# Attention and FFN on one core: batch one in a new order, its last 64 keys by two pairs, its sums in a scores bank

## The reference

```python
# q, k, v: (4, 12, 448, 64); x: (1792, 768); w_in: (768, 2048); w_out: (2048, 768); all float32
scores = cap * tanh(q @ k.T / sqrt(64) / cap)
attn = exp(scores - max(scores)); attn = attn / (sum(attn) + 1e-9)
x = (attn @ v), heads side by side            # 1792 tokens x 768
h = relu(x @ w_in); g = s * h * h + b
y = g @ w_out
```

## Time and profile before

| | |
|---|---|
| median of 3 runs | 629.79 us (629.72 to 630.93) |
| the profiled execution | 629.54 us, of which the span is 627.8 |
| busy: PE, DVE, ACT, POOL | 619.4 (99%), 332.0, 258.2, 53.9 us |
| PE in the span's 40 slices, tenths | 8 8 9 9 ... 9 8 |
| chain that ended last, by engine | PE 93%, DVE 3%, ACT 2%, issue 2% |
| KB of one load: lead (in two), q_k, v (with v_tail), w_in | 292 + 160, 448, 192 + 64, 256 |

### The profile page before, as it was taken

How to read it: one execution, slowest core, us unless ns; L and a number is a source line. 1 busy time by engine, 2 the same in 40 slices (tenths; PEclk the granted TensorE clock), 3 DMA queues, 4 the chain that set the end, 5 groups by cost and what they waited for, 6 DMA issues and landing times.

```text
span 627.8 us, 8231 instructions
## 1 busy us (share of the span) xinstructions
PE 619.4 (99%) x3230; PEld 482.7 (77%) x3230; DVE 332.0 (53%) x559; ACT 258.2 (41%) x272; POOL 53.9 (9%) x52
## 2 busy tenths in 40 slices
PE   8899999999999999999999999999999999999998
PEld 5234766667777777777779999999988888888997
DVE  2898899998677767677673233322411122111221
ACT  6885555666464646464513232222411121111220
POOL 4702624500000000000000000000000000000000
PEclk9999999999999999999999999999999999999999
DMA  8522344333322222231014211123432224111501
GB/s 264 155 89 76 109 154 149 100 97 108 105 78 100 75 87 89 73 90 58 29 45 145 75 51 51 55 69 104 152 88 67 68 94 141 48 34 33 172 2 64
DMA packets 31863, 57.17 MB, mean 91 GB/s; under 512 B 3536, under 2 KB 18000, under 8 KB 31824
## 3 DMA queue, kind: packets, MB, share of 16 engines
q1 hardware_dynamic: 31824, 56.64, 28.5%
HBM read 40.11 MB, written 16.52 MB: 90 GB/s over the span
## 4 chain that ended last, share of the span: by engine, by line
PE 93%; DVE 3%; ACT 2%; issue 2%; ACTq 0%; DVEq 0%
PE banks L465 13%; PE banks L467 13%; PE banks L466 13%; PE banks L482 12%; PE banks L483 12%; PE banks L481 12%; PE banks L423 7%; PE banks L378 5%; PE banks L337 2%; PE banks L435 1%; PE banks L403 1%; ACT e L610 1%; DVE e_sum L698 1%; PE banks L491 1%; DVE e_sum L691 1%
## 5 line engine op out<-in xcount | busy, mean ns | idle before, releaser
L465 PE MATMUL banks<-x_hi,w_hi 128*128 128x448 f32 x384 | 142.8, 372 | 0.0
L467 PE MATMUL banks<-x_hi,w_lo 128*128 128x448 f32 x384 | 140.7, 367 | 0.0
L466 PE MATMUL banks<-x_lo,w_hi 128*128 128x448 f32 x384 | 140.6, 366 | 0.0
L482 PE MATMUL banks<-x_lo,w_hi 128*128 128x512 f32 (+2 forms) x384 | 139.4, 363 | 0.0
L483 PE MATMUL banks<-x_hi,w_lo 128*128 128x512 f32 (+2 forms) x384 | 139.4, 363 | 0.0
L481 PE MATMUL banks<-x_hi,w_hi 128*128 128x512 f32 (+2 forms) x384 | 139.4, 363 | 0.0
L774 DVE SCALAR_TENSOR_TENSOR x_lo<-e,beside,x_hi 128x512 fp32r<-128x512 f32 (+1 forms) x48 | 32.5, 684 | 115.4 <-ACT x_hi L624 115.4
L465 PEld LDWEIGHTS banks<-x_hi,w_hi 128*128 128x128 f32 x384 | 72.1, 188 | 14.3 <-issue 8.3
L624 ACT ACTIVATE x_hi<-e,beside 128x512 fp32r<-128x512 f32 (+1 forms) x48 | 31.7, 669 | 116.7 <-PE banks L483 116.7
L482 PEld LDWEIGHTS banks<-x_lo,w_hi 128*128 128x128 f32 x384 | 72.1, 188 | 9.0
L481 PEld LDWEIGHTS banks<-x_hi,w_hi 128*128 128x128 f32 x384 | 72.1, 188 | 9.0
(11 more groups left out here) (62 smaller groups left out, 545.1 us busy)
## 6 DMA issues: line engine op xcount, KB each, us to landing
hidden_scratch<-hidden_sb SPq DMA_DIRECT2D x48, 224.0 KB, 1.9
beside<-q_k SPq DMA_DIRECT2D x23, 448.0 KB, 4.0
e<-hidden_scratch SPq DMA_DIRECT2D x32, 256.0 KB, 2.7
work<-w_in SPq DMA_DIRECT2D x24, 256.0 KB, 4.5
e<-w_out SPq DMA_DIRECT2D x16, 384.0 KB, 3.0
v_sb<-v SPq DMA_DIRECT2D x24, 192.0 KB, 2.5
y_t<-beside SPq DMA_DIRECT2D x10, 256.0 KB, 2.2
e<-hidden_scratch SPq DMA_DIRECT2D x16, 160.0 KB, 2.2
```

Source lines behind the costliest of these rows:

```text
L465: nc.tensor.matmul(out, w_hi[:, j, w], x_hi[:, batch % 2, c, :], start=c == 0, stop=False)
L466: nc.tensor.matmul(out, w_hi[:, j, w], x_lo[:, batch % 2, c, :], start=False, stop=False)
L467: last = nc.tensor.matmul(out, w_lo[:, j, w], x_hi[:, batch % 2, c, :], start=False, stop=c == CT - 1)
L482: nc.tensor.matmul(out, w_hi[:, j, w], ring(x_lo, n), start=False, stop=False)
```

## The change

The order of batch one changes; the later batches compute as before.

- `tail_values` takes a quad (two pairs) and runs only for odd p; `pv_done` counts quads. Even pairs are scaled one iteration later.
- `sums` writes bank 0 of the scores. It waits for `first_tanh(p + 1)` (bank 0 is read) and not for `x_done`; `values` waits for no sums. In exchange tile 0 of the scores of pair p + 2 waits for the sums to be read (`sums_read`); for even pairs tile 1 is made ahead of it.
- The first two hidden chunks of batch one go ahead of the sums of pair 5.
- DVE splits weight pieces 0 to 5, which now have six places (two in `hidden_sb`); POOL makes `x_hi` of batch one and begins with pieces 6 to 9 after it. In DVE's list `x_lo` stands apart from the scaling and mostly behind the transpose; the inversion stands behind the next pair's first add.
- SP's list has pieces 0 and 1 ahead of v, pieces 2 to 5 ahead of q and k of pair 2.
- `WARM_UP` goes from 25 to 13.

```diff
-WARM_UP = 25
+WARM_UP = 13
-        def sums_out(p):
-            return pv[:, (p + 1) % 2, 0:S]
+        def sums_out():
+            return scores[:, 0, 0:S]
         def products(p):
-            return p + 1 if p < PAIRS else PAIRS + (p - PAIRS) // 2 + 1
+            return p // 2 + 1
...
             def load_w_in(piece):
-                reach(sp, w_in_lo, piece - 3)
+                if piece >= CT:
+                    sp.wait_ge(w_in_lo, piece - CT + 1 if piece < CT + 4 else piece - 3)
...
             load_qk(1)
-            load_v(0)
             load_w_in(0)
             load_w_in(1)
+            load_v(0)
+            for piece in range(2, CT):
+                load_w_in(piece)
             load_qk(2)
-            load_w_in(2)
-            load_w_in(3)
             load_v(1)
             load_v(2)
-            load_w_in(4)
             load_qk(3)
-            load_w_in(5)
-            load_w_in(6)
+            for piece in range(CT, CT + 4):
+                load_w_in(piece)
             load_v(3)
...
-                if p <= PAIRS:
-                    for head in range(2 if p else 0):
+                if p <= PAIRS and p % 2 == 0:
+                    for head in range(2):
+                        last = row_scores(p, head, 1, 2 + head)
+                    if p > 0:
+                        pe.wait_ge(sums_read, p - 1)
+                        for head in range(2):
+                            last = row_scores(p, head, 0, head)
+                elif p <= PAIRS:
+                    reach(pe, sums_read, p - 1)
+                    for head in range(2):
                         row_scores(p, head, 0, head)
-                    if p % 2 and p > 1:
+                    if p > 1:
                         pe.wait_ge(last_read, last_group(p - 1))
...
             def values(p):
-                reach(pe, sums_read, min(p, PAIRS))
...
             def sums(p):
-                reach(pe, x_done, p)
+                pe.wait_ge(first_read, first_group(p + 1))
...
                 values(p)
-                tail_values(p, 1)
+                if p % 2:
+                    tail_values(p // 2)
                 if p % 2 and p + 1 < PAIRS:
                     pe.wait_ge(first_read, first_group(p + 1))
                     tail_scores((p + 1) // 2, 2)
+                if p + 1 == PAIRS:
+                    for c in range(2):
+                        hidden_chunk(0, c)
                 sums(p)
-            for c in range(CT - 1):
+            for c in range(2, CT - 1):
                 hidden_chunk(0, c)
             pe.wait_ge(first_read, first_group(PAIRS))
+            pe.wait_ge(sums_read, PAIRS)
...
-            add_first_e(0)
+            for piece in range(4):
+                if piece == 2:
+                    add_first_e(0)
+                w_in_high(piece)
+                w_in_low(piece)
             for p in range(PAIRS):
                 add_last_e(p)
                 if p == 0:
+                    w_in_high(4)
+                    w_in_low(4)
                     dve.wait_ge(guard_done, 2)
-                else:
-                    scale_pair(p - 1)
+                if p % 2:
+                    scale(p - 1)
+                elif p > 0:
+                    x_low(p - 1)
+                turn_first(p)
+                if p % 2:
+                    x_low(p - 1)
                 add_first_e(p + 1)
-                invert_first(p)
-            scale_pair(PAIRS - 1)
+                invert_rest(p)
+                if p == 0:
+                    w_in_high(5)
+                    w_in_low(5)
+                if p % 2:
+                    scale(p)
+            x_low(PAIRS - 1)
...
             def low(piece):
-                pool.wait_ge(w_in_hi, piece + 1)
+                pool.wait_ge(w_in_hi, max(piece + 1, CT + 4))
...
-            for piece in range(CT):
-                high(piece)
-                low(piece)
-            for piece in range(CT, CT + 4):
-                high(piece)
-
-            pool.wait_ge(x_done, PAIRS)
+            for p in range(PAIRS):
+                pool.wait_ge(x_done, p + 1)
+                nc.gpsimd.tensor_copy(x_hi[:, 0, p, :], xt[:]).then_inc(x_hi_done, 1)
+
+            pool.wait_ge(w_in_lo, CT)
+            pool.wait_ge(x_hi_done, PAIRS)
+            for piece in range(CT, CT + 4):
+                high(piece)
             for piece in range(CT, CT + 4):
                 low(piece)
```

More of the change, by code:

```diff
@@ L124, in attention_ffn @@
         v_tail_in = [sem(f"v_tail_in{i}") for i in range(2)]
-        w_in_in = [sem(f"w_in_in{i}") for i in range(4)]
+        w_in_in = [sem(f"w_in_in{i}") for i in range(CT)]
         w_out_in = [sem(f"w_out_in{i}") for i in range(W_RAW)]
@@ L209, in hidden_tile, with w_in_place, w_in_loads, w_in_raw @@
             return hidden_sb[:, n % 3, :] if n < (B - 1) * JT else work[:, n % 4, 0:S]
+        def w_in_place(piece):
+            return piece if piece < CT else (piece - CT) % 4
+        def w_in_loads(piece):
+            return 16 * (1 if piece < CT else 2 + (piece - CT) // 4)
+        def w_in_raw(piece):
+            place = w_in_place(piece)
+            raw = work[:, place, :] if place < 4 else first_raw[:, place - 4, :]
+            return raw
+        def w_in_of(tensor, piece):
+            f, c = divmod(piece, CT)
+            return tensor[:, f * JPP:(f + 1) * JPP, c * P:(c + 1) * P]
         def y_acc(c):
@@ L425, in values, with tail_values @@
                 last.then_inc(main_done, 1)
[L427 to L432, removed]
+            def tail_values(quad):
+                i = quad % 2
+                pe.wait_ge(v_tail_in[i], 16 * (quad // 2 + 1))
+                for odd in range(2):
+                    keys = slice(odd * D, (odd + 1) * D)
                     for head in range(2):
                         rows = slice(head * D, (head + 1) * D)
-                        last = nc.tensor.matmul(pv_out(p)[rows], v_tail[keys, i, head * D:(head + 1) * D],
+                        last = nc.tensor.matmul(pv_out(2 * quad + odd)[rows], v_tail[keys, i, head * D:(head + 1) * D],
                                                 e[keys, G1 + head, :], start=False, stop=True)
@@ L439, in sums @@
             def sums(p):
-                out = sums_out(p)
+                out = sums_out()
                 pe.wait_ge(e_sum_done, 3 * (p + 1))
-                reach(pe, x_done, p)
+                pe.wait_ge(first_read, first_group(p + 1))
                 for head in range(2):
@@ L682, in _, with w_in_high, w_in_low @@
         def _(dve):
+            def w_in_high(piece):
+                dve.wait_ge(w_in_in[piece], 16)
+                nc.vector.tensor_copy(w_in_of(w_hi, piece), w_in_raw(piece).rearrange("p (j n) -> p j n", n=P)
+                                      ).then_inc(w_in_hi, 1)
+            def w_in_low(piece):
+                dve.wait_ge(w_in_hi, piece + 1)
+                nc.vector.tensor_tensor(w_in_of(w_lo, piece), w_in_raw(piece).rearrange("p (j n) -> p j n", n=P),
+                                        w_in_of(w_hi, piece).bitcast(F32), ALU.subtract).then_inc(w_in_lo, 1)
             def add_first_e(p):
@@ L703, in add_last_e, with turn_first, invert_rest @@
                                         ).then_inc(e_sum_done, 1)
-            def invert_first(p):
+            def turn_first(p):
                 dve.wait_ge(sums_done, p + 1)
-                nc.vector.transpose(turned[:], sums_out(p)).then_inc(sums_read, 1)
+                nc.vector.transpose(turned[:], sums_out()).then_inc(sums_read, 1)
+            def invert_rest(p):
                 dve.wait_ge(sums_read, p + 1)
@@ L748, in split_low, with scale @@
                                         ).then_inc(qk_lo_done, 1)
-            def scale_pair(p):
+            def scale(p):
                 batch, c = divmod(p, PAIRS)
@@ L756, in scale_pair, with x_high @@
                 nc.vector.tensor_tensor(xt[:], pv_out(p), r_sum[:, p % 2, :], ALU.mult).then_inc(x_done, 1)
+            def x_high(p):
+                batch, c = divmod(p, PAIRS)
                 if batch >= 2:
@@ L761, in scale_pair, with x_low @@
                 nc.vector.tensor_copy(x_hi[:, batch % 2, c, :], xt[:]).then_inc(x_hi_done, 1)
+            def x_low(p):
+                batch, c = divmod(p, PAIRS)
                 dve.wait_ge(x_hi_done, p + 1)
@@ L764, in scale_pair @@
                                         ALU.subtract).then_inc(x_lo_done, 1)
+            def scale_pair(p):
+                scale(p)
+                x_high(p)
+                x_low(p)
             def square(n):
```

29 lines of the change are left out of this document (12 added, 17 removed).

## The result

The changed kernel takes 626.78 us (626.27 to 627.45, six executions), the kernel before 630.13 in the same comparison; the ratio is 0.9946, 95% interval 0.9934 to 0.9959. Timed again later it was 626.81 against 629.46, ratio 0.9958 (0.9943 to 0.9973). The forecast was 626.8 us, in a range of 625.6 to 628.6. The profiled execution has a span of 625.7 where the one before had 627.8, 2.1 us less; it is the longest of the six (627.45 us), whose other spans are 624.5 to 625.5.

A forecast was written before the change was run, and what follows sets the result against it. From 6.25 to 58.77 us a ring of PE, DVE and ACT binds, then PE alone; tail scores 3.0 us earlier (start and hidden chunks, less ring losses) give 629.8 - 3.0 = 626.8 us, range 625.6 to 628.6.

The forecast's parts named there:

- The walk: Step-by-step times of each pair's sums on PE, from 15.4 to 52.8 us; tail scores at 55.8, 3.0 us earlier.
- gap for the transpose: PE idle after an odd pair's sums for drain, transpose and hand-back before tile 0 of later scores: 0.97 us.
- gap for the adds: PE idle ahead of the sums of pairs 2 and 4, waiting for DVE's adds: near 0.9 us.
- the ring: Batch-one stretch where PE, DVE and ACT are almost equally loaded and wait on each other; PE busy 48.2 of 52.5 us.
- The clock: PE at 1.2 GHz until about 5.7 us, so ACT's first tanh starts at 5.8, 1.55 us earlier, not 2.45.
- The landing of piece 0: First weights piece, with 1156 instead of 1412 KB through its end, lands near 7.2 us, bounds 6.7 and 8.2.
- Collisions with POOL: POOL's x_hi cast beside DVE's adds of the next pair, for odd pairs: 0.3 us, twice; bounds 0 and 0.6.
- The two-pair product: Last 64 keys for two pairs at once: 0.9 us of PE work saved three times, 2.7 us.
- The sums' bank: Sums in bank 0 of the scores: the wait for `xt` goes, but tile-0 scores two pairs on wait for `turn_first`.
- POOL's absence: POOL idle until the first x_hi: DVE's adds cost 1.05 us rather than 1.2 to 2.1, its largest gain.
- A: The forecast itself holds: gain 2.2 to 3.8 us, time 626.0 to 627.6 us; chance 0.62.
- D: Late-landing weights pieces block DVE's in-order queue; 4 us late gives gain -0.4, time 630 to 631.2 us; chance 0.03.

The follow-up runs named there:

- e3: Changed kernel with the old order of PE and DVE in the ring and x_hi on DVE; new weights, loads and warm-up kept: 626.33 us.
- e8: Changed kernel with e7's edit and one weights piece fewer on DVE ahead of pair 0's adds: 624.67 us.
- e9: Changed kernel with SP waiting for weights piece 0 to land before issuing the load of piece 2 and all that follows: 626.66 us.
- e1: Kernel before with 13 warm-up products instead of 25, nothing else: 629.01 us.
- e10: Changed kernel with x_hi of batch one on DVE again, right behind each scaling, instead of on POOL: 627.28 us.
- e4: Changed kernel with the last 64 keys' product again for each pair, three more products on PE: 627.56 us.
- e7: Changed kernel with the small inversion steps, scaling and x_lo of odd pairs moved behind the next pair's two last adds: 625.47 us.
- e12: e3 with one weights piece fewer ahead of pair 0's adds, piece 5 going into DVE's wait in pair 4: 626.51 us.
- e11: e1 plus 18 small filler products on PE ahead of pair 1's sums, where it waits for xt: 628.90 us.

## Why the prediction was right

*The walk.* Of the mechanism these parts came as predicted: no wait for `xt`, a gap for the transpose after sums 1 and 3, a gap for the adds ahead of sums 2 and 4, a stretched add beside POOL's cast, half rate at the first scores, and no gap behind the tail scores. Predicted were 7.5, 7.7, 7.3, 7.7 and 7.2 us between the sums, measured 7.57, 7.34, 7.50, 7.35 and 7.41: single steps off by up to 0.4, the ring 40.28 where the walk had 40.4 (55.8 less 15.4). The gap for the transpose was put at 0.97 and is 0.84, that for the adds at 0.9 and is 0.6; the other steps took up to 0.2 more than the prices of step and shape gave. So the two errors cancel, and that the ring is right to 0.1 us is in part luck. The method that gave this: split each group of products into a price for the step and one for the change of shape, and follow three in-order lists at once.

*The clock.* Half rate until about 5.7, ACT's first tanh at 5.8: measured 5.93. That the moment could not be known shows e3, where the score loads behind the same 13 products take 182 to 187 ns from 3.9 us on, and ACT's first tanh starts at 5.08. The moment lay between 3.9 and 6.2 us over the profiles and moves the first tanh by up to 0.9 us (5.03 in e8, 5.93 here). The Trainium skill, "TensorE: Matmul & The Clock Gate", section "Part 1: The HAM clock gate", says that it differs from run to run, by 500 ns either way. The profiles agree that it differs, but by more: 2.3 us from the earliest to the latest.

*The landing of piece 0* is the term that was mis-sized: 7.2, bounds 6.7 and 8.2, measured 8.85. I had made it earlier with the bytes ahead of it; the old list shows no effect of those bytes, and e9 none of the loads behind it. With four pieces ahead of the adds the start then is 16.37 instead of 15.4, and that is why the profiled execution gained 2.1 and not 3.0. Where the piece landed at 7.45, in the second profile of the changed kernel, the start is 15.58 and the tail scores stand at 55.85, where the walk had 55.8: with its input right the walk comes out. Over the eleven profiles with the new loads the piece landed between 7.45 and 8.85, four times later than the upper bound of 8.2.

*The median* fell by 3.35 and 2.65 us in the two comparisons. The forecast time was hit to 0.02 us, which is luck: the 629.8 from which 3.0 was taken is the median of three executions, and the later medians of the same kernel are 629.25, 629.46 and 629.48. What the 3.35 has beyond the 2.65 lies in the kernel before. Of its 6, 23, 9 and 15 executions 3, 3, 2 and 2 take 630.4 to 631.5 us, the others 628.6 to 629.8. Where the mean granted clock of each execution is on record, in the last three groups, it is 0.997 in exactly these seven and 0.999 or 1.0 in the other forty; in all 63 executions of the changed kernel and of its variants it is 0.999 or 1.0. So the kernel before loses PE's clock somewhere in some executions, and the changed kernel did not in any. That it loses it in its wait for `xt`, as e1 does (the same kernel but for the warm-up), is likely but not shown, as none of the seven was profiled. The prediction did not reckon with this.

*Collisions with POOL* were put at 0.3 each and are 0.24 (1.32 less 1.08); e10 prices the alternative. By the Trainium skill, "SBUF — State Buffer", section "Who interferes with whom", the two can't read at once, and had the cast got in first, the add would have waited for its whole length. Here the first of the two adds (28.79 to 29.87) started ahead of the cast (28.94), and the cast took 1.35 instead of 0.56, most of it waiting, as the rule has it; the second add lost 0.24, less than the cast's 0.56.

*The two-pair product* was set down as 2.7 us less PE work, and the walk then gave nearly all of it to the new waits. e4 confirms it: 0.40 us in the ring. *The sums' bank* was said to lose from pair 1 on; e3 confirms that too. What the prediction did not say is that the change would have been as good without either: it saw that POOL's absence is the largest gain on DVE, and credited the lost wait for `xt` to the bank as well, where e3 has 0.46 of 1.88 left with the old bank.

*The rivals' sums.* The edges of A, a gain of 2.2 to 3.8, don't come out of its terms: two collisions (0.3 more or less each) and six hand-overs give 1.8 to 3.9. D is off in the same way: with 0.2 us to spare, pieces 4 us late make the gain -0.8, not -0.4. Neither changes the forecast time.

## What to carry to other kernels

In a ring of engines near 80 to 90% each, work taken from one engine turns into its wait unless the step that it waits for moves too; look at which step of the next engine stands ahead of the one that is waited for. Here three DVE steps that nobody needed soon stood ahead of the adds, and moving them behind (e7) took 1.4 us off the ring, where 2.7 us of saved products took 0.4 (e4). Before an engine is given work beside another, look for operations of the other that take twice as long at some places as at others: POOL's weights cost the ring most of 1.85 us (e3), and the new order as it stood brought nothing; with the adds first (e7, e8 against e3, e12) it is worth 0.6 to 0.9 us.

## What the runs showed of the hardware

PE's granted clock fell to 0.54 over 3.7 us after a stretch in which PE was busy 2.0 of 4 us, with 2.31 us as the longest wait (e1); in the kernel before, with a wait of 1.88 there, the profiled execution kept full rate. The mean granted clock of an execution tells the two apart without a profile: 0.997 in eight of e1's twelve executions, in none of e11's eleven, where PE is kept busy in that wait. A load issued 1 us sooner and with 256 KB less ahead of it landed no sooner (7.45 to 8.85 against 8.0 to 8.2), and holding back the loads behind it did not help either (7.80, one profile). Whoever compares two single profiles at the start of this kernel compares these two moments too: the clock's and the load's.
